# Banded attention and two feed-forward layers on one core: the global columns of two heads transposed together, with zero-padded v rows copied by DMA

## What is computed

```python
scores = scale * np.matmul(q, k.transpose(0, 1, 3, 2))     # B=2, H=8, S=768, D=64
pos = np.arange(S); rel = pos[:, None] - pos[None, :]
is_global = pos[None, :] < int(n_global)                    # n_global = 8
is_local = (rel >= 0) & (rel < int(n_local))                # n_local = 96
keep = is_global | is_local
dist = np.where(is_global & ~is_local, float(n_local), np.abs(rel))
scores = np.where(keep, scores - slopes[h] * dist, -1e9)
a = softmax(scores); attn = np.matmul(a, v)
h = x @ w_in; x2 = (h * tanh(softplus(h))) @ w_out          # x: 1536 x 512, w_in to 2048
for e in range(4):                                           # w1: 512 to 1024
    out += p[:, e:e+1] * (np.maximum(x2 @ w1[e], 0) @ w2[e])
```

## Time and profile before

| | us |
|---|---|
| median of 3 runs | 904.14 |
| lowest, highest | 903.17, 905.11 |
| the profiled execution | 902.35 |
| its span, first to last instruction | 900.5 |
| attention ends at about | 149 |

### The profile page before, as it was taken

The page is one execution under the profiler, slowest core; times in us unless marked ns, Lnnn a source line. Parts: engine busy times, 40 slices in busy tenths (PEclk is TensorE's granted clock), DMA queues, the critical chain, the costliest instruction groups (busy, mean ns, idle before and its releaser), DMA issues.

```text
span 900.5 us, 12637 instructions
## 1 busy us (share of the span) xinstructions
PE 873.6 (97%) x4916; PEld 444.9 (49%) x4916; DVE 483.3 (54%) x1010; ACT 319.2 (35%) x597; POOL 257.6 (29%) x218
## 2 busy tenths in 40 slices
PE   6888999999999999999999999999999999999998
PEld 6666876444444444444444444444444444444443
DVE  7756887999999989874542125222134322212121
ACT  4898886545555656552021110102010111101020
POOL 1278993222222222210029200077000292000000
PEclk9987999999999999999999999999999999999999
DMA  9871420000000000202000500001300000000001
GB/s 214 276 237 37 142 84 1 1 1 1 1 7 3 1 1 1 97 1 94 10 1 0 186 1 1 6 0 53 134 1 6 0 0 0 1 24 23 35 12 49
DMA packets 52004, 39.19 MB, mean 44 GB/s; under 512 B 40816, under 2 KB 41712, under 8 KB 51440
## 3 DMA queue, kind: packets, MB, share of 16 engines
q1 hardware_dynamic: 49888, 34.31, 12.5%
q10 hardware_dynamic: 2064, 4.19, 1.3%
HBM read 35.35 MB, written 3.15 MB: 43 GB/s over the span
## 4 chain that ended last, share of the span: by engine, by line
PE 89%; ACT 5%; DVE 4%; issue 1%; POOL 0%; DVEq 0%
PE bank L607 67%; PE bank L676 14%; PE bank L546 2%; PE bank L578 2%; ACT scaled L865 2%; PE bank L597 2%; ACT tmp L849 1%; ACT tmp L890 1%; PE bank L501 1%; DVE xT L1213 1%; PE bank L559 1%; DVE tmp L1117 1%; ACT hid L839 0%; DVE tmp L1228 0%; DVE tmp L1346 0%
## 5 line engine op out<-in xcount | busy, mean ns | idle before, releaser
L961 ACT ACTIVATE hid<-bank 128x512 f16<-128x512 f32 x96 | 57.3, 597 | 422.2 <-PE bank L607 422.2
L607 PE MATMUL bank<-xT,wA 128*128 128x512 f16 (+1 forms) x864 | 194.6, 379 | 0.0
L1337 DVE SCALAR_TENSOR_TENSOR hid<-bank,hid 128x512 f16<-128x512 f32 x96 | 66.4, 691 | 181.8 <-ACT hid L961 181.8
L607 PEld LDWEIGHTS bank<-xT,wA 128*128 128x128 f16 x864 | 84.5, 98 | 100.6
L676 PE MATMUL bank<-hid,wB 128*128 128x512 f16 x576 | 132.2, 379 | 0.9 <-DVE xT L1213 0.9
L607 PE MATMUL bank<-xT,wB 128*128 x576 | 125.3, 379 | 0.0
L607 PE MATMUL bank<-wA,hid 128*128 128x512 f16 x576 | 125.3, 379 | 0.0
L607 PE MATMUL bank<-wB,hid 128*128 128x512 f16 x576 | 125.3, 379 | 0.0
L815 POOL TENSOR_TENSOR tmp<-tmp 128x512 f32<-128x512 f32 x48 | 61.4, 1280 | 190.2 <-DVE tmp L1360 190.2
L770 POOL TENSOR_SCALAR stage<-stage,sc 128x1024 f32<-128x1024 f32 x32 | 36.0, 1124 | 256.7 <-DVEq L1330 250.4
L1417 DVE SCALAR_TENSOR_TENSOR acc<-bank,pg,acc 128x512 f32<-128x512 f32 x36 | 27.0, 750 | 131.7 <-PE bank L607 131.7
(11 more groups left out here) (111 smaller groups left out, 948.8 us busy)
## 6 DMA issues: line engine op xcount, KB each, us to landing
stage<-in_moe_w SPq DMA_DIRECT2D x8, 2048.0 KB, 9.8
stage<-in_moe_w_in SPq DMA_DIRECT2D x1, 4096.0 KB, 16.6
wB<-in_moe_w_out ACTq DMA_DIRECT2D x1, 4096.0 KB, 16.3
hid<-in_q SPq DMA_DIRECT2D x16, 192.0 KB, 3.4
hid<-in_k SPq DMA_DIRECT2D x16, 192.0 KB, 3.5
xT<-in_v SPq DMA_DIRECT2D x8, 384.0 KB, 5.0
out_y<-acc SPq DMA_DIRECT2D x12, 256.0 KB, 2.0
rows<-max SPq DMA_DIRECT2D x4, 128.0 KB, 4.1
```

Of the source, the lines that this page charges most:

```text
L607: last = pe.matmul(dst, lhs(c, a), rhs(c, b), start=(c == 0 and n == 0), stop=(c == chunks - 1 and n == 2))
L961: act.activation(hv[:, f, 0, :], psum(f % 4), ACT.Relu).then_inc(f_hi, 1)
L1337: dve.scalar_tensor_tensor(hv[:, f, 1, :], psum(f % 4), 0.0, hv[:, f, 0, :], ALU.max, ALU.subtract).then_inc(f_ready, 1)
```

## The change

- The global columns of the two heads of a far tile now lie side by side. Both units share one buffer (`s_two`, 2 x 288 columns): the even unit has the order tile before, own tile, global; the odd unit has global first. The 128 columns from 256 on then hold 32 global columns of the even unit, 32 of the odd one and 64 of the odd unit's band.
- `turn` makes two transposes for an even far unit, and three for an odd one, whose third takes the 128 shared columns. The eviction of an even far unit is 256 columns wide, that of an odd one 384.
- `pv` takes the third block from the odd unit's transposed P for both heads. The other operand is `vg`: for each head 128 rows, in which only the 32 rows of that head hold v and the others are zero. `vg` is zeroed once by VectorE at the start; for each pair ScalarE issues two transfers at step 2 (`load_globals`) that copy 32 rows of v, high and low parts, within SBUF. `pv(4)` waits for them.
- `pv` runs three steps behind `turn` instead of two (`PV_LAG`), since an even unit needs the odd one's transposed block; there are four `pT_b` buffers. VectorE's `output` steps move back by one step.
- The odd unit's distances stand in another order: ScalarE copies a second table at the start, 32 and 256 columns.
- Three zeroing instructions over 96 columns go away.

```diff
+    W = BAND_W[2]
+
+    def far(u):
+
+        return u // 2 >= 2
+
+    def unit_blocks(u):
+
+        blks = band[u // 2]
+        return blks[-1:] + blks[:-1] if far(u) and u % 2 else blks
+
+    def table_at(u):
+
+        return BAND_COLS if far(u) and u % 2 else BAND_AT[u // 2]
...
+        vg = scratch(4 * VD).bitcast(F16).rearrange("p (b s a d) -> p b s a d", b=2, s=2, a=2)
...
-        W = 3 * P
-        dist_b, key_b = (scratch(BAND_COLS) for _ in range(2))
-        s_b = [scratch(W) for _ in range(3)]
-        pT_b = [scratch(W).bitcast(F16).rearrange("p (s n) -> p s n", s=2) for _ in range(3)]
+        dist_b, key_b = scratch(BAND_COLS + W), scratch(BAND_COLS)
+        s_two = [scratch(2 * W) for _ in range(2)]
+        pT_b = [scratch((2 + n % 2) * P).bitcast(F16).rearrange("p (s n) -> p s n", s=2) for n in range(4)]
...
+        PV_LAG = 3
...
+        def unit_cols(u, banded):
+
+            return offsets(unit_blocks(u) if banded else full[u // 2])[1]
+
+        def s_b(u):
+
+            at = W * (u % 2)
+            return s_two[u // 2 % 2][:, at:at + unit_cols(u, True)]
+
         def p_out(u, banded):
 
             if not banded:
                 return bank[2][:, 0:S], pT_g
-            n = len(band[u // 2]) * P
-            return psum(4 + u % 2, n), pT_b[u % 3][:, :, 0:n]
+            n = P * ((2 + u % 2) if far(u) else len(band[u // 2]))
+            return psum(4 + u % 2, n), pT_b[u % 4][:, :, 0:n]
...
+                runs.sort(key=lambda run: -run[1])
...
-                src = s_b[u % 3] if banded else s_g
...
+                if banded and far(u):
+                    two = s_two[u // 2 % 2]
+                    start = W + GLOBAL_COLS if u % 2 else 0
+                    for b in range(2):
+                        last = pe.transpose(dst[:, b * P:(b + 1) * P], two[:, start + b * P:start + (b + 1) * P], ident[:])
+                    if u % 2:
+                        last = pe.transpose(dst[:, 2 * P:3 * P],
+                                            two[:, W - GLOBAL_COLS:W - GLOBAL_COLS + P], ident[:])
+                else:
+                    src = s_b(u) if banded else s_g
+                    for b in range(len((band if banded else full)[u // 2])):
+                        last = pe.transpose(dst[:, b * P:(b + 1) * P], src[:, b * P:(b + 1) * P], ident[:])
...
             def pv(i, slot, u, banded):
 
                 m = 2 * i + slot
                 qt, a = u // 2, u % 2
-                pe.wait_ge(pT_act, UNITS * m + u + 1)
-                pe.wait_ge(pT_dve, UNITS * m + u + 1)
+                shared = banded and far(u)
+                needs = u + 1 - u % 2 if shared else u
+                pe.wait_ge(pT_act, UNITS * m + needs + 1)
+                pe.wait_ge(pT_dve, UNITS * m + needs + 1)
                 if u == 0:
                     pe.wait_ge(v_split, m + 1)
+                if shared and u == 4:
+                    pe.wait_ge(vg_in, 32 * (m + 1))
                 if u in (0, UNITS // 2):
 
                     pe.wait_ge(o_ready, 2 * m + 1 + u // (UNITS // 2))
                 _, pt = p_out(u, banded)
-                keys = [kt for kt, _ in (band if banded else full)[qt]]
+                keys = [(kt, b) for b, (kt, n) in enumerate((band if banded else full)[qt]) if n == P]
                 dst = psum(6 + u // (UNITS // 2), VD, (u % (UNITS // 2)) * VD)
-                for b, kt in enumerate(keys):
+                parts = [(pt[:, :, b * P:(b + 1) * P], v_parts(m)[:, :, a, kt]) for kt, b in keys]
+                if shared:
+                    parts.append((pT_b[(u + 1 - a) % 4][:, :, 2 * P:3 * P], vg[:, slot, :, a]))
+                for b, (p_b, v_b) in enumerate(parts):
                     for n, (x, y) in enumerate(((0, 0), (0, 1), (1, 0))):
-                        last = pe.matmul(dst, pt[:, x, b * P:(b + 1) * P], v_parts(m)[:, y, a, kt],
-                                         start=(b == 0 and n == 0), stop=(b == len(keys) - 1 and n == 2))
+                        last = pe.matmul(dst, p_b[:, x], v_b[:, y],
+                                         start=(b == 0 and n == 0), stop=(b == len(parts) - 1 and n == 2))
                 last.then_inc(pv_done, 1)
...
-                        ahead, behind = reach(i, slot, u, 3), reach(i, slot, u, -2)
+                        ahead, behind = reach(i, slot, u, 3), reach(i, slot, u, -PV_LAG)
                         if ahead and u % 2:
                             scores_of_two(*ahead)
+                        if not after(i, slot) and u == UNITS - 1:
+                            pv(*behind, banded)
+                            pv(i, slot, UNITS - 3, banded)
+                            behind = None
...
+                    near = BAND_COLS - GLOBAL_COLS
+                    act.copy(dist_b[:, BAND_COLS:BAND_COLS + GLOBAL_COLS], dist_b[:, near:BAND_COLS])
+                    act.copy(dist_b[:, BAND_COLS + GLOBAL_COLS:BAND_COLS + W],
+                             dist_b[:, near - 2 * P:near]).then_inc(second_table, 1)
...
+                    if banded and u == 2:
+                        load_globals(i, slot)
...
+            def load_globals(i, slot):
+
+                m = 2 * i + slot
+                act.wait_ge(v_split, m + 1)
+                if m == 0:
+                    act.wait_ge(vg_zero, 1)
+                for a in range(2):
+                    act.dma_start(vg[a * GLOBAL_COLS:(a + 1) * GLOBAL_COLS, slot, :, a],
+                                  v_parts(m)[0:GLOBAL_COLS, :, a, 0]).then_inc(vg_in, 16)
...
+            dve.memset(vg, 0.0).then_inc(vg_zero, 1)
...
-            for s in s_b:
-                last = dve.memset(s[:, 2 * P + GLOBAL_COLS:3 * P], 0.0)
-            link(last)
...
+                    if m == 0 and u == 5:
+                        dve.wait_ge(second_table, 1)
...
-            OUTPUT_AT = UNITS // 2 + 2
+            OUTPUT_AT = UNITS // 2 + PV_LAG
...
-                    if banded and 1 <= u < 4 and before(i, slot):
-                        output(*before(i, slot), 1, u - 1)
+                    at = u - PV_LAG + 1
+                    if banded and 0 <= at < 3 and before(i, slot):
+                        output(*before(i, slot), 1, at)
```

More of the change, by code:

```diff
@@ L236, in program @@
         v_pairs_max = sem("v_pairs_max")
+        vg_zero, vg_in = sem("vg_zero"), sem("vg_in")
+        second_table = sem("second_table")
         band_ready = sem("band_ready")
@@ L512, in score_parts @@
             def score_parts(i, slot, u, banded):
-                blks = (band if banded else full)[u // 2]
+                blks = unit_blocks(u) if banded else full[u // 2]
                 qt, a = u // 2, u % 2
@@ L576, in turn @@
                     pe.wait_ge(pT_dve, at - 1)
-                for b in range(len((band if banded else full)[u // 2])):
-                    last = pe.transpose(dst[:, b * P:(b + 1) * P], src[:, b * P:(b + 1) * P], ident[:])
+                if banded and far(u):
[10 more added lines that the diff above has]
+                        last = pe.transpose(dst[:, b * P:(b + 1) * P], src[:, b * P:(b + 1) * P], ident[:])
                 last.then_inc(pT_psum, 1)
@@ L846, in expo @@
                 act.wait_ge(s_ready, PB * i + UNITS * slot + u + 1)
-                width = offsets((band if banded else full)[u // 2])[1]
-                t = (s_b[u % 3] if banded else s_g)[:, 0:width]
+                t = s_b(u) if banded else s_g
                 act.activation(t, t, ACT.Exp, bias=nmax[:, u:u + 1], scale=-1.0).then_inc(p_ready, 1)
@@ L1040, in _ @@
             dve.wait_ge(iotas, 3)
-            dve.scalar_tensor_tensor(rel_b, rel_b, -1.0e9, rel_b, ALU.mult, ALU.max)
-            for s in s_b:
-                last = dve.memset(s[:, 2 * P + GLOBAL_COLS:3 * P], 0.0)
-            link(last)
+            link(dve.scalar_tensor_tensor(rel_b, rel_b, -1.0e9, rel_b, ALU.mult, ALU.max))
             dve.wait_ge(bounds_in, 32)
@@ L1094, in band_tables @@
                 link(dve.tensor_scalar(rel_b, rel_b, bf[:, 1:2], -1.0 / SCALE, ALU.min, ALU.mult))
-                dve.tensor_tensor(dist_b, rel_b, key_b, ALU.add).then_inc(band_ready, 1)
+                dve.tensor_tensor(rel_b, rel_b, key_b, ALU.add).then_inc(band_ready, 1)
             def full_tables(link):
@@ L1112, in biased @@
                 m = 2 * i + slot
-                width = offsets((band if banded else full)[qt])[1]
                 if banded:
+                    width = unit_cols(u, banded)
+                    if m == 0 and u == 5:
+                        dve.wait_ge(second_table, 1)
                     dve.wait_ge(s_psum, UNITS * m + u + 1)
                     dve.sem_inc(carrier, 1)
-                    dve.tensor_tensor_reduce(s_b[u % 3][:, 0:width], psum(u % 3, width),
-                                             dist_b[:, BAND_AT[qt]:BAND_AT[qt] + width],
+                    dve.tensor_tensor_reduce(s_b(u), psum(u % 3, width),
+                                             dist_b[:, table_at(u):table_at(u) + width],
```

2 lines of the change are left out of this document (1 added, 1 removed).

## The result

The changed kernel takes 906.64 us (median of 20 runs, 903.97 to 909.92), the kernel before 904.73 beside it (median of 20, 902.35 to 905.32 but for one slow run of 933.98, which the ratio leaves out). Ratio 1.0027, 95% interval 1.0019 to 1.0036; it is formed from means, and the quotient of the medians is 1.0021. The forecast was 900.6, range 897.5 to 904.2: the sign was wrong and the time lies outside the range. The profiled execution of after took 906.1, span 904.3. The one of before, 902.35, is the fastest of its 20, so the two profiles differ by more (3.8 us) than the kernels do.

The account below looks back on a forecast made before the run. TensorE bounds most pairs, ScalarE parts of pairs 1 to 3. Pairs 4-6 -1.86, 1 and 7 -1.24, 2 and 3 -0.56, 0 -0.3, start +0.4: -3.56, so 900.6 us, range 897.5 to 904.2.

Parts of the forecast that it names:

- Pairs 4 to 7, the saving: Fewer transposes and narrower evictions: 1.86 us gained in pairs 4 to 6, plus 0.48 and 0.28 in pair 7.
- the reciprocals: VectorE's border burst: an added reciprocal of six columns costs about 0.1 us a pair, estimated from a memset's 0.12.
- The issues: ScalarE, pairs 2 and 3: one issue hides, the second costs about 0.4 us a pair, 0.8 together; elsewhere nothing.
- The border: Between pairs: reordering looks like 0.46 us gained, given nothing because TensorE's scores wait for `biased` behind all of VectorE's burst.
- later `pv` waits less: Rival where all reordering counts: pairs 4 to 6 give 1.08 us each, later `pv` 0.6 more; 898.6, chance 0.16.
- VectorE keeps the border: Rival: VectorE's burst decides, pairs 4 to 6 give 0.14 us each; with both issues counting, 903.0; chance 0.14.
- The transfers' landing: Copies before `pv(4)` land in 3.3 us, bound 7.5, within 5.2 us of room in pair 5, so they hide.
- the rival said of pairs 1 and 5: Copies beside the big loads land late, `pv(4)` waits 2.3 us in each of these pairs; 905.1, chance 0.07.
- the two rules that the prediction named: Copies' landing: transfers below 512 B are read, modified and written, so slower; engines alternate queues by packet, so little held back.
- The start: Zeroing `vg` on VectorE ahead of `ident`, on which TensorE's first matmul waits, costs 0.4 us.
- Pair 7: End of attention: 9 of 27 `pv` matmuls move ahead of the last early product, 0.28 us gained besides 0.48 for transposes.

Follow-up runs that it names:

- x_short_even: Kernel before, with even far units transposing and evicting two blocks instead of three, block 1 standing in for the third in `pv`; ratio 0.9960, 900.96 us.
- x_no_copies: Changed kernel without the two transfers of each pair and without the wait for them; ratio 0.9988, 902.90 us.
- x_one_copy: Changed kernel with only one of the two transfers of each pair, the even heads'; ratio 0.9995, 903.75 us.
- x_split_pool: Changed kernel with GpSimd copying the v rows and `pv` two steps behind, the even unit's shared block multiplied with the odd unit's; ratio 0.9968, 901.34 us.
- x_pool_copies: Changed kernel with the v rows copied by GpSimd's own instructions instead of ScalarE's transfers, lag three kept; ratio 0.9990, 903.91 us.
- x_pool_output: Changed kernel with GpSimd copying the v rows and the last output step one step sooner, lag three kept; ratio 0.9993, 902.62 us.
- x_issue_idle: Changed kernel with both issues moved from step 2 to step 10 of the pair before, those of pair 0 staying; ratio 1.0042, 907.16 us.
- x_sp_copies: Changed kernel with the transfers of pairs 2 to 7 issued by SyncE into a slot for each pair, pairs 0 and 1 staying with ScalarE; ratio 1.0012, 904.42 us.
- x_before_lag3: Kernel before, with `pv` three units behind, a fourth `pT_b` and the output steps one unit later; ratio 1.0037, 906.92 us.
- x_split_pv: Changed kernel with `pv` two steps behind, the even unit's shared block multiplied with the odd unit's, ScalarE's copies kept; ratio 1.0026, 906.61 us.

## Why the prediction was wrong

- **Pairs 4 to 7, the saving (-2.62 by the sum, 1.86 + 0.48 + 0.28): right.** x_short_even has -2.48. It keeps the old order, so the 0.28 and the reciprocals (0.10 each) aren't in it, and by the sum's own terms it should have -2.64. A reciprocal takes 0.18 in after, not 0.1.
- **The issues, the step that failed most.** I took 0.4 for the second issue of each pair, from the 0.42 of L922, and let it count in pairs 2 and 3 only, 0.8 in all, "nothing in the pairs where ScalarE has gaps". Measured: 0.61 each, up to 1.3, and a price in the pairs taken as free. After less x_no_copies is 0.57 in pair 4, 1.06 in pair 5 (0.73 of it the wait for the landing) and 1.09 in pairs 6 and 7, 2.72 on the ruler and 3.5 us in all. The half-right part was that one issue hides (x_one_copy). The error in reasoning was the busy share: 12.30 of 14.40 says that ScalarE has 2.1 us free in a pair, not that they lie where the issues stand. At step 2 `expo`, eviction and copy out follow each other without a gap and TensorE waits for the last of them.
- **The border.** I wrote that `biased` of unit 2 stands behind all of the burst either way, and took the new order at a reciprocal. But L1157 was ahead of L1213, where its time was partly covered, and comes behind the eviction of unit 11, where it is on the path. The row of the scores at 119.17, which the prediction names, is this one of the chain of before:

```profile
119.17 0.84 PE bank L546 x6
```

  On the kernel before the new order costs 1.53 on the ruler and 3.4 us in all; in the changed kernel, from x_split_pool to x_pool_copies, 1.25 and 2.0. The place of L1157 is 0.96 of the first and 0.34 of the second. The rest is the lag of three itself, in part a wait for ScalarE's copy out (x_pool_output), in part not found; the prediction had no term for it, and from "later `pv` waits less" it even expected a gain in one of its rivals. The first rival, "VectorE keeps the border", had the place and the burst right but gave it 1.4 us less gain instead of a loss of its own.
- **The transfers' landing.** The room was 5.2 us, the value taken 3.3 and the bound 7.5; measured 1.8 to 6.6. In pair 5, beside w1's load, `pv(4)` waited once, as the rival said of pairs 1 and 5; pair 1 waited for none. The chain of after has it as one piece:

```profile
109.16 6.64 DMA hid<-xT
```

  and TensorE's timeline has the wait:

```profile
115.93 0.34 PE L640 MATMUL bank<-xT,tmp 128*128 128x65 f16 x6 [0.73 <-DMA hid<-xT]
```

  The Trainium skill ("DMA: Bandwidth & Descriptors", section "Queues, rings and completion order") would have a small transfer pass beside a bulk load packet by packet; here the same transfer took 6.6 beside the load and 2.9 at the median. The changed kernel issues w1's load at 107.33, ahead of pair 5's copies at 108.51 and 109.16, which land after 5.9 and 6.6; in pairs 3, 4 and 6, with no load beside them, they take 1.8 to 1.9. In x_issue_idle the same copies of pair 5 are issued at 105.18 and 105.82, ahead of the load, and land after 1.8 and 1.9:

```profile
DMA to landing us min/median/max: 1.8/1.9/1.9
...
106.64 0.37 SPq L480 DMA_DIRECT2D stage<-in_moe_w  x1
```

  x_sp_copies has its six issued ahead of the load at 1.8 to 2.5. So the copies that land late are those issued behind a bulk load that is still under way; by which of the two rules that the prediction named, no run shows. 0.73 of it reached TensorE.
- **The start (+0.4): wrong, harmless.** VectorE's `vg` memset takes 0.28, and `ident` comes at 3.09, 0.06 later than in the earlier trace rows; TensorE's first matmul starts 0.01 later.
- **Pair 7 (-0.28 for the earlier `pv`).** Not seen apart: from the turn of x's chunks to the last early product x_no_copies has 12.36 against 12.52 before, where 0.76 was forecast for all of the pair.
- **The sum on the ruler:** -2.48 for the saving, +1.53 for lag and output steps (x_before_lag3), +2.72 for the issues and the wait (after less x_no_copies) is +1.77, measured +1.67. What this tests is the first two, -0.95 against the -1.05 of x_no_copies; the third is by its making the distance from there to after. In whole time x_short_even stands at -3.6, x_no_copies 2.5 above it, after 3.5 above that: +2.4. The lag alone, on the kernel before, took 3.4 where this leaves it 2.5, and the intervals are about 1 us to each side. The steps above are enough for the miss, but how it divides between them depends on what else is in the kernel: beside lag two the issues cost 3.52 on the ruler (x_split_pv less x_split_pool), beside lag three 2.72. The pairs before the ruler can't be split further, because single executions differ there by more than the parts.

## What to carry to other kernels

Price a transfer by the time its issue holds the engine at the place where it stands, for each one, and ask whether that engine's gaps there are room or a link of a chain: a busy share can't tell. Here two issues in a row cost where one hid, and GpSimd, which copied 32 rows in 0.29 us in time that it had, did the same with no cost on the ruler. When an instruction is moved past one that another engine's wait hangs on, its whole length can change sides: follow it from the cover that it leaves to the release that it now precedes.

## What the hardware showed that I had not expected

- An issue of a small strided transfer (32 partitions, pieces of 130 B) held ScalarE for 0.59 to 0.64 us in all but two of after's 16 (SyncE for 585 ns at the least), where w_out's 4 MB took 0.42 and the maxima's 0.34; single ones took 1.31 (after, pair 7), 1.67 (x_issue_idle) and on SyncE 2.24 (x_sp_copies), for no reason that a run shows.
- Small transfers landed after 1.8 to 1.9 us in pairs 3, 4 and 6 of after, after 2.6 to 4.0 in pairs 0, 1 and 7, after 5.0 to 6.6 with w_out's or w1's load already under way (pairs 2 and 5), and 11.3 at the most in x_issue_idle (pair 2, beside w_out).
- 26 matmuls of filler kept the granted clock at 1.00 between 32 and 40 us, where it was 0.59 and 0.56 without them, and the kernel was not measurably faster for it.
